# Multiplying the identity into unread PSUM columns at TensorE's waits

## The chip, the cores and the metric

The kernel runs on one core of one Trainium2 chip. The metric is the device time of that core in microseconds, the median of several runs. TensorE (PE in the profile) multiplies, VectorE (DVE), ScalarE (ACT) and GpSimd (POOL) work on SBUF and, except POOL, read PSUM; SyncE (SP) issues most of the DMAs. Each engine runs its own instruction stream in order, and they meet at semaphores. The profiler records the share of its full clock that TensorE was granted: 1.00 is 2.4 GHz, 0.50 is 1.2 GHz.

## The reference

Three parts follow each other. A delta-rule attention over 768 steps for 4 x 8 heads of 48 dimensions; a mixture of 8 experts with a greedy, capacity-bound assignment of 3072 tokens (each expert takes 384); and a dense feed-forward block with 2048 hidden units.

```python
for t in range(S):                                    # attention
    y[:, :, t] = einsum('bhd,bhde->bhe', q[:, :, t], state)
    v_old = einsum('bhde,bhd->bhe', state, kt)
    state = state + bt * einsum('bhd,bhe->bhde', kt, vt - v_old)
...
for idx in argsort(-(x @ w_gate).flatten()):          # routing
    tok, e = idx // E, idx % E
    if assigned[tok] < 0 and counts[e] < N // E: assigned[tok] = e; counts[e] += 1
...
out[mask_e] = relu(x[mask_e] @ w1[e]) @ w2[e]          # experts
h = out @ w_in;  y = (h * sigmoid(h)) @ w_out          # dense block
```

## The kernel before

Three blocks of instructions run one after the other, with a meeting of all engines between them: `constants` (identity and triangle), `attention`, `experts`.

`attention` goes through 24 tiles `n` of 128 rows (two chunks of 64 steps for 8 heads). Within a tile the triangular system is solved by a doubling scheme: `turn_k` transposes the keys, `products` forms key-key and query-key products, `level2`, `level4`, `level8` and `prod8`, `prod24` form powers of the triangle and their sum, `correct` and `apply` (three and two times) refine the right side, `read_state`, `to_state` and `outputs` exchange with the running state, and `turn_x` and `gate` transpose the output and multiply it by the gate's weights to give the routing logits. The order on TensorE is written out by hand and mixes tile `n` with `level*` and `products` of tile `n + 1` and `n + 2` and with `outputs`, `turn_x`, `gate` of tile `n - 1`. The first tile has nothing of a tile before it to mix in, and the last two tiles have less of the tiles behind them. Between these steps ScalarE and VectorE take the results out of PSUM, and GpSimd scales keys and values (`scale_k`, `scale_v`) and builds `LP` and `Hm` from the identity and the products (`unit`).

GpSimd's order matters here: `scale_k(2)`, `scale_v(2)`, and only then `unit(1)`, whose result `P1_ok` the second half of `level4(1)` waits for. `scale_v(2)` waits for the load of `v_in` for tile 2. SyncE issues that load after the two loads of 3 MB for `w_in` and `w_out`.

`experts` routes in 8 rounds. The first round has no other work to hide behind. VectorE searches the threshold in 8 steps of 4 bits (`search_digits`); in each of them TensorE counts with 24 small products (L1259), VectorE compares, TensorE spreads the hits with one product (L1262), and VectorE picks the next digit. Then `place(0, 0)` forms prefix sums, `place(0, 1..4)` turn one-hot tiles into the list of tokens, GpSimd gathers the tokens' rows of `x_rows` with three indirect DMAs, and TensorE transposes them (L1393). From there on TensorE runs the products of the experts and the dense block (`one_pass`, L1272), and the searches of the later rounds are put between them at fixed numbers of passes (L1235).

Of the kernel before, what the change touches and what calls it, by code (L numbers as in the profile page):

```python
# [14 lines left out]
C = 128  # L15
# [14 lines left out]
def by_tile(w):  # L30

    return w[:, :, :].rearrange("p a b -> p (a b)").rearrange("p (k f) -> p k f", k=KD)


def whole_and_rest(nc, sb, whole, rest, shape):
# [6 lines left out]
def attention(nc, k_t, v_t, q_t, beta_t, wg, x_rows, logits, identf, up_f, rc, PS, wi, wo, w_in, w_in_hi, w_in_lo, w_out, w_out_hi, w_out_lo):  # L42

    ctx = ExitStack()
    with ctx:
# [502 lines left out]
        def _(pe):  # L548
# [14 lines left out]
            def turn_k(n):  # L563
                pe.wait_ge(kb_ok, n + 1)
                if n:
                    pe.wait_ge(kT_sb, n)
                if n >= 2:
                    pe.wait_ge(P8_sb, n - 1)
                for i in range(HG):
                    last = nc.tensor.transpose(PS[:, 2, i * C:i * C + C], K[n % 3][:, i, :, :].rearrange("p r d -> p (r d)"), identf[:, :])  # L570
                last.then_inc(kT_ps, 1)
# [110 lines left out]
            def gate(n):  # L682
# [4 lines left out]
                    last = mm(PS[:, 7, DM:DM + E], xT[:, k, :], wg_sb[:, k, :], start=(k == 0), stop=(k == KD - 1))  # L687
                last.then_inc(lg_ps, 1)

            pe.wait_ge(mask_ok, 8)  # L690
            turn_k(0)
            products(0)
            turn_k(1)
            level2(0)
            level4(0)
            level8(0)
            products(1)
            prod8(0)
            for n in range(NT):
                nxt = n + 1 < NT  # L700
                from_state(n)
                if n:
                    outputs(n - 1)
                prod24(n)
                if n + 2 < NT:
                    turn_k(n + 2)
                correct(n, 0)
                if n:
                    turn_x(n - 1)
                apply(n, 0)  # L710
                if nxt:
                    level2(n + 1)
                correct(n, 1)
                if n:
                    gate(n - 1)
                apply(n, 1)
                if nxt:
                    level4(n + 1)
                read_state(n)
                correct(n, 2)  # L720
                if nxt:
                    level8(n + 1)
                to_state(n)
                if n + 2 < NT:
                    products(n + 2)
                if nxt:
                    prod8(n + 1)
            outputs(NT - 1)
            turn_x(NT - 1)
            gate(NT - 1)  # L730


BITS = 31
# [2 lines left out]
DIGITS = 8  # L736
# [84 lines left out]
def experts(nc, x_rows, w1, w2, w_in_hi, w_in_lo, w_out_hi, w_out_lo, out, logits, identf, up_f, rc, PS):  # L821
# [3 lines left out]
    with ctx:  # L825
# [402 lines left out]
        def _(pe):  # L1228
# [25 lines left out]
            def digits():  # L1254
                for i in range(DIGITS):
                    c0 = 0 if i == DIGITS - 1 else 1
                    pe.wait_ge(over_ok, i + 1)
                    for m in range(NT):
                        last = mm(PS[0:CANDS - c0, 3, 0:E], over[:, m, c0:CANDS], onehot[:, m, :], start=(m == 0), stop=(m == NT - 1))  # L1259
                    last.then_inc(over_ps, 1)  # L1260
                    pe.wait_ge(hits_ok, i + 1)
                    mm(PS[:, 4, 0:E], ones_b[0:CANDS - c0, :], hits[0:CANDS - c0, :], start=True, stop=True).then_inc(hits_ps, 1)  # L1262

            PLACES = 1 + NT // HOT
            AT = [17 * i + 5 * min(i, PARTS) for i in range(COUNTS)]
# [73 lines left out]
            def turn(k):  # L1339
# [26 lines left out]
                for f in range(KF2 + LAG):  # L1366
# [10 lines left out]
                    if h >= 0:  # L1377
# [6 lines left out]
                        for j in range(MT_TOK):  # L1384
                            fourth(k, j, h, 1)

            digits()
            for i in range(PLACES):
                place(0, i)
            for j in range(MT_TOK):  # L1390
                pe.wait_ge(x_ld[j], 16)
                for d in range(KD):
                    last = nc.tensor.transpose(PS[:, bank_of(("T", 0, d)), j * C:j * C + C], xg[:, j, d * C:d * C + C], identf[:, :])  # L1393
                    if j == MT_TOK - 1:
                        last.then_inc(filled, 1)
# [65 lines left out]
```

## Time and profile before

| | |
|---|---|
| median of 3 runs | 1082.27 us (1079.34 to 1089.83) |
| the profiled execution's own time | 1078.51 us |
| its span in the trace | 1076.7 us |
| PE busy (matmul) | 962.6 us, 89% of the span |
| DVE, ACT, POOL busy | 729.9, 412.4, 471.7 us |
| granted TensorE clock, mean of the records | 0.95 |

The profile is of one execution. Busy time is the time in which an engine had an instruction under way. The span is what the trace covers; the time is what the device reports for the whole launch. The granted clock has no record ahead of about 40 us in this trace, and the views show 1.00 there; the durations of the matmuls show the clock then.

### The profile page before, as it was taken

How to read it: one execution, taken by the hardware profiler on the slowest of the kernel's cores; microseconds unless marked ns; L12 is line 12 of the kernel's file. 1: busy time of each engine (PE TensorE's matmuls, PEld its weight loads, DVE VectorE, ACT ScalarE, POOL GpSimd, SP SyncE). 2: the span in 40 equal slices, each digit the busy share in tenths (PEclk: the TensorE clock that was granted, in tenths of full speed). 3: DMA queues.
4: the chain of work that ended last, by engine and by line, in shares of the span. 5: the costliest groups of instructions: out<-in, count | busy, mean ns of one | idle time of the engine just before them, and what ended most of it. 6: DMA issues, size and time to landing. Idle time of an engine off the chain costs nothing.

```text
span 1076.7 us, 32107 instructions
## 1 busy us (share of the span) xinstructions
PE 962.6 (89%) x13967; PEld 897.1 (83%) x13967; DVE 729.9 (68%) x1572; ACT 412.4 (38%) x930; POOL 471.7 (44%) x583
## 2 busy tenths in 40 slices
PE   4888889898888539989988999999999999999996
PEld 3777778887777429889987899899899899899996
DVE  5667676767665388887778788788788788783000
ACT  3444443444443034234334326326326326326321
POOL 3235545555550024345434445535535535535532
PEclk9999998999997559999998999999999999999998
DMA  8322222111110030030040030030030030030000
GB/s 294 124 70 59 66 52 59 48 48 48 47 49 18 9 139 1 1 139 23 1 140 16 9 125 23 15 126 23 15 120 28 16 118 23 23 117 23 23 1 22
DMA packets 31563, 61.93 MB, mean 58 GB/s; under 512 B 3776, under 2 KB 23360, under 8 KB 31040
## 3 DMA queue, kind: packets, MB, share of 16 engines
q1 hardware_dynamic: 28352, 50.45, 14.5%
q0 software_dynamic: 3072, 9.44, 2.7%
q8 instruction: 110, 1.80, 0.7%
q14 instruction: 29, 0.24, 0.1%
HBM read 50.44 MB, written 9.44 MB: 56 GB/s over the span
## 4 chain that ended last, share of the span: by engine, by line
PE 49%; DVE 14%; issue 1%; POOL 1%; DMA 1%; ACT 0%; DVEq 0%
PE PS L1272 47%; DVE above L1075 3%; DVE cand L1104 3%; DVE cs L1079 2%; DVE w_lo L1218 2%; PE PS L1235 1%; DVE delta L1086 1%; DMA xg<-x_rows,idx 1%; PE PS L1259 1%; PE PS L1290 1%; DVE weighed L1083 0%; DVE over L1120 0%; POOL xg L959 0%; PE PS L1250 0%; DVE w_lo L1214 0%
## 5 line engine op out<-in xcount | busy, mean ns | idle before, releaser
L952 POOL TENSOR_TENSOR act_t<-whole,act_t 128x384 fp32r<-128x384 f32 x192 | 210.6, 1100 | 303.7 <-ACT whole L1010 302.9
L1004 ACT ACTIVATE act_t<-PS 128x384 fp32r<-128x384 f32 x192 | 94.6, 492 | 376.4 <-PE PS L1272 376.4
L1272 PE MATMUL PS<-w_out_hi,act_t 128*128 128x384 f32 x768 | 222.7, 346 | 1.6 <-POOL act_t L952 1.6
L1272 PE MATMUL PS<-x2T,w_in_hi 128*128 128x384 f32 x768 | 223.3, 345 | 0.1
L1272 PEld LDWEIGHTS PS<-x2T,w_in_hi 128*128 128x128 f32 x768 | 142.2, 191 | 3.5 <-POOL x2T L952 2.0
L1272 PEld LDWEIGHTS PS<-w_out_hi,act_t 128*128 128x128 f32 x768 | 142.2, 190 | 1.9 <-POOL act_t L952 1.9
L1272 PE MATMUL PS<-w_out_lo,act_t 128*128 128x384 f32 x384 | 133.0, 346 | 0.0
L1272 PE MATMUL PS<-x2T,w_in_lo 128*128 128x384 f32 x384 | 132.0, 344 | 0.0
L1272 PE MATMUL PS<-xgT,w_hi 128*128 128x384 f32 x384 | 110.1, 346 | 0.6 <-ACT whole L1008 0.6
L1272 PE MATMUL PS<-act_t,w_hi 128*128 128x384 f32 x384 | 106.4, 337 | 0.0
L1075 DVE TENSOR_TENSOR above<-V,cand 128x576 bf16<-128x576 f32 x112 | 91.7, 818 | 3.9
L1010 ACT ACTIVATE whole<-PS 128x384 f32<-128x384 f32 x192 | 93.5, 487 | 0.0
L1079 DVE TENSOR_REDUCE cs<-above 128x24 bf16<-128x576 bf16 (+1 forms) x119 | 86.8, 730 | 4.1
L1272 PEld LDWEIGHTS PS<-w_out_lo,act_t 128*128 128x128 f32 x384 | 73.0, 190 | 0.0
L1272 PEld LDWEIGHTS PS<-x2T,w_in_lo 128*128 128x128 f32 x384 | 72.9, 190 | 0.0
L1272 PEld LDWEIGHTS PS<-xgT,w_hi 128*128 128x128 f32 x384 | 71.6, 192 | 1.3 <-DVE w_lo L1214 0.9
L1272 PEld LDWEIGHTS PS<-act_t,w_hi 128*128 128x128 f32 x384 | 69.9, 188 | 0.1
L1272 PE MATMUL PS<-xgT,w_lo 128*128 128x384 f32 x192 | 66.2, 345 | 0.0
L1272 PE MATMUL PS<-act_t,w_lo 128*128 128x384 f32 x192 | 64.9, 338 | 0.0
L656 PE MATMUL PS<-X,Hm 64*64 64x48 f32 x1536 | 61.9, 236 | 1.5 <-ACT X L303 1.1
L237 POOL TENSOR_TENSOR vs<-v_in,sqb_all 128x384 f32<-128x384 f32 x24 | 19.9, 831 | 96.6 <-DVE Bv L455 82.6
L959 POOL DMA_INDIRECT xg<-x_rows,idx x24 | 26.7, 1111 | 80.7 <-DVE idx L1211 77.9
(204 smaller groups left out, 1848.6 us busy)
## 6 DMA issues: line engine op xcount, KB each, us to landing
w_sb<-moe_w SPq DMA_DIRECT2D x16, 1536.0 KB, 8.2
k_in<-k_t SPq DMA_DIRECT2D x24, 192.0 KB, 4.2
KQ<-q_t SPq DMA_DIRECT2D x48, 96.0 KB, 2.2
v_in<-v_t SPq DMA_DIRECT2D x24, 192.0 KB, 3.1
x_rows<-ysb SPq DMA_DIRECT2D x48, 96.0 KB, 2.2
w_in<-moe_w_in SPq DMA_DIRECT2D x1, 3072.0 KB, 11.8
w_out<-moe_w_out SPq DMA_DIRECT2D x1, 3072.0 KB, 20.1
xg<-x_rows,idx POOLq DMA_INDIRECT x24, 3.1
```

Of the source, the lines that this page charges most:

```text
L237: nc.gpsimd.tensor_tensor(by_head(vs[p][:, :]), by_head(v_in[p][:, :]), sqb_all[:, n, :].unsqueeze(2).to_broadcast([C, H, D]), ALU.mult).t ...
L656: each(lambda h, b: mm(PS[rows(b), 6, col(h)], Hm[n % 2][rows(b), h, :], X[n % 2][rows(b), col(h)], start=True, stop=True)).then_inc(HX_ps, 1)
L952: nc.gpsimd.tensor_tensor(lo, whole_of(t), hi.bitcast(F32), ALU.subtract).then_inc(rest_ok, 1)
L959: nc.gpsimd.indirect_dma_start(out=xg[:, j, :], out_offset=None, in_=x_rows, in_offset=bass.IndirectOffsetOnAxis(ap=idx[k % 2][:, j:j + 1] ...
L1004: nc.scalar.activation(hi, src, func).then_inc(hi_ok, 1)
L1010: nc.scalar.activation(whole_of(t), src, func).then_inc(whole_ok, 1)
L1075: chain(v.tensor_tensor(above[:, 0:cands, :, :].rearrange("p c e m -> p c (e m)"), flat.unsqueeze(1).to_broadcast([C, cands, E * NT]), t.u ...
L1079: v.tensor_reduce(cs[:, 0:cands, :], above[:, 0:cands, :, :], AX.X, ALU.add).then_inc(cs_ok, 1)
L1086: chain(v.tensor_reduce(o, weighed[:, :, :].rearrange("p c e -> p (c e)"), AX.X, ALU.max))
L1104: v.tensor_scalar(cand[:, :], pair_i[:, i + 1, :], cur[:, 0:1], delta[:, 0:1], ALU.bitwise_xor, ALU.bitwise_xor).then_inc(dv, 1)
L1218: v.tensor_tensor(w2_part(w2_lo, q), w2_part(w2_sb, q), w2_part(w2_hi, q).bitcast(F32), ALU.subtract).then_inc(w2_split, 1)
L1272: ins = mm(o, a, b, start=start, stop=stop, skip_group_check=True)
```

## The change

`keep_busy` multiplies the identity (128 x 128, fp32) by itself into the last 128 columns of a PSUM bank, columns that nothing reads at those points. In the attention it is called with bank 5 ahead of and within the first tile, with bank 2 in the last two tiles; in the experts with bank 2 in the first routing round. No semaphore is signalled and no wait is added, and every call stands on TensorE alone, ahead of the wait of the step that follows it.

```diff
+def keep_busy(nc, PS, identf, bank, times):
+    for _ in range(times):
+        nc.tensor.matmul(PS[:, bank, 512 - C:512], identf[:, :], identf[:, :], start=True, stop=True, skip_group_check=True)
...
+            keep(5, 22)
             pe.wait_ge(mask_ok, 8)
             turn_k(0)
+            keep(5, 3)
             products(0)
             turn_k(1)
+            keep(5, 8)
             level2(0)
+            keep(5, 4)
             level4(0)
+            keep(5, 4)
             level8(0)
...
+                if n == 0:
+                    keep(5, 4)
                 prod24(n)
                 if n + 2 < NT:
                     turn_k(n + 2)
+                else:
+                    keep(2, 4)
                 correct(n, 0)
...
                 if nxt:
                     level2(n + 1)
+                else:
+                    keep(2, 3)
                 correct(n, 1)
...
                 correct(n, 2)
                 if nxt:
                     level8(n + 1)
+                else:
+                    keep(2, 2)
                 to_state(n)
...
             outputs(NT - 1)
+            keep(2, 2)
             turn_x(NT - 1)
+            keep(2, 2)
             gate(NT - 1)
+            keep(2, 6)
...  (experts; keep is keep_busy on bank 2)
                     mm(PS[:, 4, 0:E], ones_b[0:CANDS - c0, :], hits[0:CANDS - c0, :], ...).then_inc(hits_ps, 1)
+                    keep(4 if i < DIGITS - 1 else 13)
...
+            keep(10)
             digits()
             for i in range(PLACES):
                 place(0, i)
+                keep(13 if i == 0 else 2 if i < PLACES - 1 else 20)
```

## Rows read from the trace of the kernel before

**Rows 1.** The page: shares of the chain that ended last, by engine.

```profile
PE 49%; DVE 14%; issue 1%; POOL 1%; DMA 1%; ACT 0%; DVEq 0%
```

**Rows 2.** Stretches: us, busy us (instructions) of PE, PEld, DVE, ACT, POOL, clock, DMA share, GB/s.

```profile
330.60:340.80 10.20, 10.01 (x235) 9.71 (x237) 5.02 (x17) 3.79 (x11) 2.49 (x2) 0.50 0.02 4
...
347.60:360.10 12.50, 10.50 (x175) 9.51 (x175) 1.12 (x3) 2.23 (x6) 0.00 (x0) 0.50 0.07 17
360.10:396.50 36.40, 9.02 (x226) 7.10 (x226) 24.48 (x90) 4.90 (x9) 2.67 (x3) 0.50 0.26 94
396.50:405.70 9.20, 7.75 (x25) 5.95 (x26) 8.09 (x16) 4.95 (x11) 3.82 (x5) 0.50 0.13 40
```

**Rows 3.** TensorE in order of time, tiles 0 and 1: start, us, instructions.

```profile
10.87 1.08 PE L570 MATMUL PS<-identf,K 128*128 128x128 f32 x4 [10.87 <-POOL K L227]
...
36.72 0.94 PE L602 MATMUL PS<-LP,L 64*64 64x128 f16 x14
...
41.84 0.66 PE L627 MATMUL PS<-St,KQ 48*64 48x48 f32 x30
```

**Rows 4.** TensorE, tiles 21 to 23: first at clock 1.00, from 330.6 at 0.50.

```profile
316.85 0.52 PE L679 MATMUL PS<-identf,ysb 128*128 128x128 f32 x3
317.35 1.14 PE L656 MATMUL PS<-X,Hm 64*64 64x48 f32 x32
...
319.65 0.83 PE L687 MATMUL PS<-wg_sb,xT 128*128 128x8 f32 x6
...
321.64 0.56 PE L602 MATMUL PS<-LP,L 64*64 64x128 f16 x14
...
326.06 0.64 PE L627 MATMUL PS<-St,KQ 48*64 48x48 f32 x29
...
329.68 0.43 PE L647 MATMUL PS<-rb,P 64*64 64x48 bf16 x16 [0.83 <-issue]
...
330.69 1.94 PE L656 MATMUL PS<-X,Hm 64*64 64x48 f32 x32
...
342.19 0.68 PE L627 MATMUL PS<-St,KQ 48*64 48x48 f32 x32
```

**Rows 5.** One line's instructions: matmuls of turn_k, ns min/median/max.

```profile
L570 PE MATMUL PS<-identf,K x96: 272/273/473, 10.9 to 315.8; 128*128 128x128 f32 x96
```

**Rows 6.** GpSimd in order of time, behind the load of v_in for tile 2.

```profile
34.47 0.83 POOL L237 TENSOR_TENSOR vs<-v_in,sqb_all 128x384 f32<-128x384 f32 x1 [13.96 <-DMA v_in<-v_t]
35.25 1.27 POOL L246 TENSOR_TENSOR LP<-eye,GP 128x512 f16<-128x512 f32 x1
```

**Rows 7.** TensorE in the last tile, then ScalarE at the block's end.

```profile
347.66 0.62 PE L647 MATMUL PS<-rb,P 64*64 64x48 bf16 x16 [0.66 <-DVE rb L452]
348.21 1.45 PE L687 MATMUL PS<-wg_sb,xT 128*128 128x8 f32 x6
...
354.66 1.91 PE L671 MATMUL PS<-X,GP 64*64 64x48 f32 x32
...
360.11 0.34 ACT L339 COPY logits<-PS 64x8 f32<-64x8 f32 x2 [1.54 <-PE PS L687]
```

**Rows 8.** TensorE in the first routing round.

```profile
376.22 0.75 PE L1259 MATMUL PS<-onehot,over 128*15 128x8 bf16 x24 [1.22 <-DVE over L1120]
...
385.42 0.22 PE L1243 MATMUL PS<-GQ,tri 128*128 128x48 f16 x1 [3.19 <-DVE GQ L1177]
...
396.53 0.90 PE L1393 MATMUL PS<-identf,xg 128*128 128x128 f32 x3 [4.76 <-DMA xg<-x_rows,idx]
```

**Rows 9.** GpSimd at the first expert's start.

```profile
400.64 2.92 POOL L952 TENSOR_TENSOR xgT<-whole,xgT 128x384 fp32r<-128x384 f32 x3 [3.65 <-ACT whole L1008]
```

**Rows 10.** Stretches with waits and one behind a wait, columns as in Rows 2.

```profile
475.00:480.00 5.00, 2.00 (x12) 1.51 (x11) 4.86 (x6) 1.11 (x3) 3.10 (x4) 1.00 0.28 79
...
480.70:484.20 3.50, 3.50 (x13) 3.50 (x12) 3.43 (x5) 1.39 (x2) 1.67 (x1) 0.51 0.00 0
...
555.00:560.00 5.00, 3.44 (x25) 2.96 (x24) 3.96 (x9) 2.32 (x4) 3.08 (x4) 1.00 0.16 49
```

More of the change, by code:

```diff
@@ L688, in gate, with keep @@
                 last.then_inc(lg_ps, 1)
+            def keep(bank, times):
+                keep_busy(nc, PS, identf, bank, times)
+            keep(5, 22)
             pe.wait_ge(mask_ok, 8)
             turn_k(0)
+            keep(5, 3)
             products(0)
             turn_k(1)
+            keep(5, 8)
             level2(0)
+            keep(5, 4)
             level4(0)
+            keep(5, 4)
             level8(0)
@@ L1262, in digits, with keep @@
                     mm(PS[:, 4, 0:E], ones_b[0:CANDS - c0, :], hits[0:CANDS - c0, :], start=True, stop=True).then_inc(hits_ps, 1)
+                    keep(4 if i < DIGITS - 1 else 13)
+            def keep(times):
+                keep_busy(nc, PS, identf, 2, times)
             PLACES = 1 + NT // HOT
```

## The prediction

> **What bounds the kernel now.** I read the page first. Half of the chain that ended last is TensorE [rows 1], so its clock matters. The stretch view places the low clock: in this execution it lies at 0.50 from 330.6 to 340.8 and again from 347.6 to 405.7 us, that is in the last two tiles of the attention, in the whole first routing round and at the first expert's start [rows 2]. Short dips at tiles 8 to 18 are not touched by the change. The start is low too: the four transposes at 10.87 take 1.08 us [rows 3], while three take 0.52 at full clock [rows 4] and 0.90 at the low one [rows 8], and the longest of its line takes 0.47 us against a median of 0.27 [rows 5]. So it is at the low level too. In these three regions TensorE alternates between work that the clock halves and waits that it doesn't. So the reader must look, wait by wait, at two things: what a full clock saves, and whether the added products fit into the wait.
>
> **The price of one added product.** The trace has no 128 x 128 fp32 product of 128 columns. Two rows make it up. An fp32 product leaves two matmul records (three gate products are six records [rows 4]); a transpose, one record of the same shape, starts every (0.52 - 0.27) / 2 = 0.12 us at full and (0.90 - 0.47) / 2 = 0.21 us at low clock [rows 4, 5, 8], where 0.27 and 0.47 are one record's duration at each. So one call is 0.25 us at full and 0.43 us at low clock. If a plain product's record took half a transpose's, a call would be 0.12; if weight loads didn't overlap, twice the 0.25. I take 0.25 and 0.43. Everything below is what a block costs beyond the wait that it stands in.
>
> **The first tile: 0.** 22 calls start at about 2.4 us and end at 11.8 us if the clock never rises, 0.9 us after the key tile that TensorE waits for at 10.87 [rows 3]; with a rise on the way they fit. In either case it doesn't matter. What counts is the next thing that is late. GpSimd scales the values of tile 2 only at 34.47, after 13.96 us of waiting for a load that stood behind the two 3 MB loads, and builds LP of tile 1 behind that, from 35.25 to 36.52 [rows 6]; the second half of level4(1) starts at 36.72 [rows 3]. This path of DMAs doesn't know TensorE's clock. A full clock would bring TensorE to that point earlier, by about 4 us (the stretch to 36.72 is about 4.6 us of halved work), where it would wait until 36.5 all the same. Behind it, from 36.72 to from_state(1) at 41.84 are 5.12 us [rows 3], and the same steps in tile 21 take 326.06 - 321.64 = 4.42 us [rows 4]: 0.7 us are to be had, if the clock is still high after those 4 us without any product in them. Where TensorE waited for gathers (475 to 480), the clock was 0.50 right behind it [rows 10]. So I take 0, between 0.8 gained and 0.7 lost (if it now rises later than it did).
>
> **Tile 22: -2.6 us.** The four calls behind prod24(22) stand in the 0.83 us ahead of the product at 329.68 [rows 4], and the clock was at 0.50 right behind that [rows 2]. They take 0.98 us, so 0.15 too many. If they hold the clock, the stretch from apply(22, 0) to from_state(23), now 342.19 - 330.69 = 11.50 us, takes what it took a tile earlier at full clock, 326.06 - 317.35 = 8.71 us [rows 4]. That is 2.8 less 0.15. Whether the clock would have fallen there at all differs between executions; this sum is for the profiled one.
>
> **Tile 23: -2.9 us.** From the gate product at 348.21 to the end of outputs at 356.57 [rows 7] lie, at the low level, one gate (1.45 against 0.83 at full), one apply (about 1.95 against 1.14), read_state (1.1 against 0.6), one correct (0.6 against 0.4), to_state and outputs (2.8 against 1.7 together): 3.2 us less at full clock [rows 4, 7]. The 4, 3 and 2 calls ahead of the corrections and to_state are 0.98, 0.74 and 0.49 us against waits of about 0.83 (as in tile 22 [rows 4]), 0.66 [rows 7] and 0.57 us: 0.3 over. Behind outputs nothing more is won: the last output tile, copied by 357.1, must be stored by two DMAs (0.5 us each to issue, 2.2 to land), which is about 360.4, as late as the logits' copy at 360.11 to 360.45 [rows 7]. So the last 2, 2 and 6 calls (2.5 us) lie beside that store, and cost nothing unless the clock is low (then about 2).
>
> **Digits and places: +4.5 us.** Here TensorE's own work hardly depends on the clock: it waits for the end of VectorE's small steps. The gain from a full clock is at most some hundredths of a microsecond in each of 17 products. The price depends on the level. In each round TensorE waits 1.22 us between the spreading product and the next count [rows 8]. Four calls take 0.98 us at full clock, inside; at the low level 1.71, which is 0.45 to 0.5 over. Does the clock hold? The four calls are 0.98 in 2.40 us, and the 24 products of 8 columns beside them didn't lift it in the whole stretch before, though PE was busy a quarter of it [rows 2]. The nearest rows: 2.00 us of full-size work in 5 was followed by 0.50, 3.44 in 5 was not [rows 10]. 0.98 in 2.40 is 2.0 in 5, the first of them. So I take a fall in the second round, after which the share can't recover: five rounds at 0.45, or 2.2 us. The 13 calls behind the last digit are then 5.5 us in a wait of 3.19 [rows 8]: 2.1 over, since the clock rises only late in such an unbroken block. The next 13 (3.2 us) and the pairs (0.49) stand in waits for VectorE's one-hot tiles of about their own length, and the last 20 are 4.9 us against 4.76 [rows 8]; at full clock I take 0.2 for all of them. At a clock that holds, the sum of this part is -0.2; at one that never rises +13.
>
> **The first expert: -1.3 us.** The long block of 20 calls ends where the first gathered rows arrive. If the clock is high then, the last three transposes are 0.4 us shorter; but the first pass group still ends behind GpSimd's third difference, 400.64 + 2.92 = 403.56 [rows 9], so there only about 0.5 us are won. Behind it passes go at 0.17 instead of 0.32 us until 405.7, about 9 of them, 1.4 us more. The transposes leave TensorE half idle, and the clock can fall once more for a few microseconds: the ends are 0.3 and 2.0.
>
> **Sum.** 0 - 2.6 - 2.9 + 4.5 - 1.3 = -2.3 us on the profiled 1078.51 us: 1076.2. The four times shown, this one among them, have their middle at (1079.34 + 1082.27) / 2 = 1080.8, 2.3 us above the profiled one, since the executions differ in where the clock falls; the calls take away one of these places. I forecast 1077.5 us.
>
> **Rivals.**
> (a) *The calls hold the clock through the digits.* Then the part is -0.2 rather than +4.5, and the first expert keeps its 2.0: 1078.51 - 7.7 = 1070.8, with the same offset 1072. For it: no wait over 0.3 us would be left anywhere from tile 22 to the gathers. Against it: the share of busy time [rows 10]. The Trainium skill, "TensorE: Matmul & The Clock Gate", section "Why this matters for your kernels", advises to leave no long idle gaps between bursts; by that rule the digits stay fast and this rival is the outcome. The trace doesn't quite agree with the gaps as the measure: the clock fell at 330.6 behind a gap of 0.83 us [rows 4]. Chance 0.22.
> (b) *The calls run at the low clock and stand in the way, slower than before.* If the four calls in tile 22 and those in tile 23 don't hold the clock, the tiles win nothing and pay 0.9 + 0.9 + 0.6 + 0.3, the end of the block about 2, the digits 7 x 0.48 = 3.4 and 2.3, the places about 1, less 1 at the expert: some +9, so 1088 to 1090. It decides from the point where a call costs 0.43 instead of 0.25 in the digit rounds while the tiles gain nothing. Chance 0.1.
> (c) *The change does nothing.* The clock isn't moved by these products (no row of the trace shows it moved by any such), but they are shorter than I price them and fit into the waits: 1079 to 1082. Chance 0.13.
> (d) *More instructions.* Some 130 calls are about 520 more instructions for TensorE, and the trace shows stalls that nothing explains ("issue"), 1% of the chain [rows 1]. A new one of 1 to 2 us in a tile would take half of the forecast's gain; it stays within the range. Chance 0.05; the rest, 0.5, is the forecast.
>
> **How the numbers follow.** The forecast alone spans 1073 to 1081 (its unknown ends: 1.5 at the start, 1.7 at the expert, 3 in the digits, and the spread of executions). To hold 8 in 10 the range must take in most of (a) and of (c) and part of (b): 1069 to 1087. A change of 1%, about what a measurement of this kernel can tell from none, is 10.8 us. Faster by that needs less than 1071.5, half of (a) and a tail of the forecast: 0.12. Slower by that needs over 1093, a tail of (b): 0.03. Within 1%: 0.85.
>
> **What would show it.** Right: matmuls of tile 0 at full-clock durations, and yet level4(1)'s second half near 36.6 us behind the same DMA; clock 1.00 from tile 22 on, with from_state(23) 8.7 us behind apply(22, 0); digit rounds of 2.4 us while the clock is high and 2.8 to 2.9 after it has fallen; the wait for GQ gone; clock 1.00 at the first transposes. Wrong: digit rounds of 2.35 us at clock 1.00 throughout (rival a); a record of the added products over 0.2 us apart at full clock; or a shorter start, if the load of tile 2's values isn't what ends the wait there.

## The result and the profile after

| | before | after |
|---|---|---|
| median, 20 runs each | 1082.78 us | 1090.01 us |
| lowest and highest | 1078.69, 1089.83 | 1081.55, 1101.33 |
| the profiled execution's own time | 1078.51 us | 1092.40 us |
| its span | 1076.7 us | 1090.7 us |
| PE busy | 962.6 us | 1006.1 us |

The ratio after to before, both run in turn on one chip, is 1.0053, with a 95% interval of 1.0031 to 1.0074: about 5.8 us slower (0.0053 x 1082.78). This leaves out the run of 1101.33 us, which fell into a slower state, and goes by all other runs, so it differs from the 7.2 us between the two medians. I had forecast 1077.5 us and a range up to 1087, so the time lies outside the range.

The shares of the chain that ended last are the same percentages as before [rows 1], although TensorE is busy for 43.5 us more. Some of that fills waits, and some of it is a longer run at the low clock. The page of after, its chain by engine:

```profile
PE 49%; DVE 14%; POOL 1%; issue 1%; DMA 1%; ACT 0%; DVEq 0%
```

I cut both profiles at the same instructions; where one stage ends the next begins. All in us, to a tenth:

| stage | before | after | forecast change |
|---|---|---|---|
| start to from_state(1) | 41.8 | 43.4 | 0 |
| from_state(1) to from_state(22) | 284.2 | 298.0 | none made |
| tile 22 | 16.2 | 12.2 | -2.6 |
| tile 23 to VectorE's first routing step | 18.6 | 15.6 | -2.9 |
| routing to the first expert product | 39.9 | 44.8 | +4.5 |
| first 48 expert products of 384 columns | 11.1 | 12.7 | -1.3 |
| the rest | 665.0 | 664.0 | none made |

Two things stand out. The five stages that I had summed come to +1.1 us in these two profiles (+1.6 - 4.0 - 3.0 + 4.9 + 1.6) instead of -2.3. And 13.8 of the 14.0 us by which the two spans differ lie in tiles 1 to 21, where the change adds nothing.

**The start.** TensorE in after's trace in order of time (start, duration, instructions, and in brackets the idle time before them with its releaser), to be read beside [rows 3]:

```profile
2.45 6.72 PE L38 MATMUL PS<-identf 128*128 128x128 f32 x44 [2.45 <-PEq L1433]
10.95 0.63 PE L576 MATMUL PS<-identf,K 128*128 128x128 f32 x4 [1.77 <-POOL K L233]
...
37.13 0.96 PE L608 MATMUL PS<-LP,L 64*64 64x128 f16 x14 [4.10 <-POOL LP L252]
...
43.43 0.66 PE L633 MATMUL PS<-St,KQ 48*64 48x48 f32 x30
```

The 44 records (22 calls) are over at 9.2, the four transposes take 0.63 us instead of 1.08, and TensorE is early, as forecast. It then waits 4.10 us for LP. GpSimd gives that at the same point as before [rows 6]:

```profile
35.02 0.83 POOL L243 TENSOR_TENSOR vs<-v_in,sqb_all 128x384 f32<-128x384 f32 x1 [15.17 <-DMA v_in<-v_t]
35.81 1.26 POOL L252 TENSOR_TENSOR LP<-eye,GP 128x512 f16<-128x512 f32 x1
```

GpSimd goes on 0.55 us later (35.02 against 34.47), and the clock is low behind the wait, so 43.43 stands against 41.84.

**Tiles 22 and 23.** The stretch that was at 0.50 [rows 2, 4] is at full clock, and the meeting of the engines comes 0.30 us behind the last added product. TensorE in order of time, then the stretch view (from:to, us, busy us and instructions of PE, PEld, DVE, ACT and POOL, granted clock, DMA share, GB/s):

```profile
355.39 1.16 PE L38 MATMUL PS<-identf 128*128 128x128 f32 x8
356.48 0.43 PE L653 MATMUL PS<-rb,P 64*64 64x48 bf16 x16
...
366.64 0.84 PE L693 MATMUL PS<-wg_sb,xT 128*128 128x8 f32 x6
367.33 1.58 PE L38 MATMUL PS<-identf 128*128 128x128 f32 x12
369.21 2.47 PE L38 MATMUL PS<-identf 128*128 128x128 f32 x20 [0.30 <-PEq L51]
```

```profile
353.60:369.20 15.60, 14.89 (x344) 13.41 (x345) 3.93 (x7) 3.99 (x12) 0.00 (x0) 1.00 0.12 28
369.20:377.80 8.60, 6.85 (x100) 6.05 (x101) 5.47 (x21) 0.20 (x1) 0.00 (x0) 1.00 0.01 3
377.80:398.30 20.50, 19.01 (x202) 17.21 (x198) 8.93 (x39) 0.00 (x0) 0.00 (x0) 0.50 0.02 3
```

**Digits.** The last two of these stretches are the first routing round. The clock holds to 377.8 and then lies at 0.50 for 20.5 us. TensorE in order of time:

```profile
375.06 0.75 PE L1284 MATMUL PS<-onehot,over 128*15 128x8 bf16 x24 [0.64 <-DVE over L1145]
376.06 0.17 PE L1287 MATMUL PS<-hits,ones_b 15*128 15x8 bf16 x1 [0.25 <-DVE hits L1149]
376.17 1.16 PE L38 MATMUL PS<-identf 128*128 128x128 f32 x8
377.45 0.75 PE L1284 MATMUL PS<-onehot,over 128*15 128x8 bf16 x24
378.45 0.18 PE L1287 MATMUL PS<-hits,ones_b 15*128 15x8 bf16 x1 [0.25 <-DVE hits L1149]
378.56 2.08 PE L38 MATMUL PS<-identf 128*128 128x128 f32 x8
380.57 0.75 PE L1284 MATMUL PS<-onehot,over 128*15 128x8 bf16 x24
381.57 0.18 PE L1287 MATMUL PS<-hits,ones_b 15*128 15x8 bf16 x1 [0.25 <-DVE hits L1149]
381.68 2.08 PE L38 MATMUL PS<-identf 128*128 128x128 f32 x8
383.69 0.75 PE L1284 MATMUL PS<-onehot,over 128*15 128x8 bf16 x24
...
394.16 5.12 PE L38 MATMUL PS<-identf 128*128 128x128 f32 x26
```

The same four calls (8 records) take 1.16 us at full and 2.08 at the low clock. A round, from one count to the next, is 377.45 - 375.06 = 2.39 us at full clock and 3.12 at the low one (380.57 to 383.69). The count itself, 24 products of 8 columns, takes 0.75 at both: it doesn't know the clock. And at the low clock the wait for VectorE's `over`, which was 1.22 us [rows 8], is gone: the added products are now what the count waits for. Between the meeting and the fall at 377.8 no idle time of TensorE is longer than 0.64 us.

**The first expert.** The clock rises at 398.3, at the end of the 13 calls behind the last digit, and holds through the places. But the gathers then come one by one, and it falls once more at 415.3:

```profile
411.52 0.55 PE L1424 MATMUL PS<-identf,xg 128*128 128x128 f32 x3 [0.73 <-DMA xg<-x_rows,idx]
412.68 0.55 PE L1424 MATMUL PS<-identf,xg 128*128 128x128 f32 x3 [0.61 <-DMA xg<-x_rows,idx]
```

```profile
411.90:415.30 3.40, 1.72 (x11) 0.97 (x9) 3.21 (x5) 2.26 (x6) 1.31 (x2) 1.00 0.05 19
415.30:422.20 6.90, 6.63 (x21) 5.97 (x22) 3.98 (x9) 1.88 (x5) 3.90 (x4) 0.51 0.00 0
```

### The profile page after: what moved, and what is told of

Read it like the earlier page. It is cut to its first block, busy times and chain, and to the rows that moved or that the text cites. A ratio compares the mean times of both kernels' runs of the same rounds, so it can differ in the third digit from the quotient of the medians.

```text
span 1090.7 us, 32739 instructions
## 1 busy us (share of the span) xinstructions
PE 1006.1 (92%) x14283; PEld 938.6 (86%) x14283; DVE 729.1 (67%) x1572; ACT 412.8 (38%) x930; POOL 472.5 (43%) x583
## 4 chain that ended last, share of the span: by engine, by line
PE 49%; DVE 14%; POOL 1%; issue 1%; DMA 1%; ACT 0%; DVEq 0%
PE PS L1301 46%; DVE above L1100 3%; DVE cand L1129 3%; DVE cs L1104 2%; DVE w_lo L1243 2%; PE PS L38 1%; PE PS L1260 1%; DVE delta L1111 1%; DMA xg<-x_rows,idx 1%; PE PS L1284 1%; PE PS L1319 1%; DVE weighed L1108 0%; POOL xg L984 0%; PE PS L1275 0%; DVE w_lo L1239 0%
## 5 line engine op out<-in xcount | busy, mean ns | idle before, releaser
L662 PEld LDWEIGHTS PS<-X,Hm 64*64 64x64 f32 x1536 | 56.4, 152 | 8.4 <-ACT X L309 7.3
```

The costliest lines, as they stand in the source:

```text
L662: each(lambda h, b: mm(PS[rows(b), 6, col(h)], Hm[n % 2][rows(b), h, :], X[n % 2][rows(b), col(h)], start=True, stop=True)).then_inc(HX_ps, 1)
```

## The experiments

There were four studies, each with its own runs of the kernel before on the same chip, whose medians were 1085.35, 1081.53, 1077.78 and 1084.28 us. Times are compared within a study only, by the ratio given with its 95% interval. "Profiled" stages are those of the table above.

### One region at a time (first study)

**e1_front**: before with the 45 calls around the first tile alone.

```diff
 before
+            keep(5, 22)
...
+                if n == 0:
+                    keep(5, 4)
```

> Only the 45 calls in and ahead of the first tile; the last tiles and the routing are as before. Theory A (the start costs): TensorE waits some 4 us for LP of tile 1, the clock falls in that wait and comes back 3 us later than it did, so from_state(1) is 1 to 2 us late, and the 180 instructions more move the places at which the instruction stream stalls in tiles 1 to 21, which costs up to 3 us more: 1.5 to 4.5 us over before. Rival B (the start only moves work inside a wait): within 1 us of before, and the loss of the whole change lies in the routing.

Measured 1087.37 us, ratio 1.0006 (0.9976 to 1.0036): no change that can be told, so rival B's outcome and not the loss of theory A. from_state(1) came at 42.7 instead of 41.8. Tile 22, in which this kernel has no call, took 11.8 us, since the clock did not fall there; the 4.0 us that after gains in it are thus not shown to be the calls' work.

**e2_tail**: before with the calls of tiles 22 and 23 and behind the last outputs alone (`keep(2, ...)` in the attention).

```diff
 before
+                else:
+                    keep(2, 4)
...
+            gate(NT - 1)
+            keep(2, 6)
```

> Only the 23 calls in the last two tiles and behind outputs. Both theories: the clock holds at 1.00 from tile 22 to the end of the attention, and the time is 3 to 5 us under before; digit rounds of 2.40 us. If the calls at the end stand in the way of the meeting of the engines, about 1 us of it is lost.

Measured 1083.17 us, ratio 0.9993 (0.9961 to 1.0024). In the profile tiles 22 and 23 are 2.0 and 3.0 us shorter (14.2 and 15.6), as their clock is high; in the median of 12 runs only 0.8 us of that is seen, with an interval of 3.4 us to either side. The 3 to 5 us that I had expected here did not come.

**e3_routing**: before with the calls of the first routing round alone.

```diff
 before
+                    keep(4 if i < DIGITS - 1 else 13)
...
+            keep(10)
             digits()
             for i in range(PLACES):
                 place(0, i)
+                keep(13 if i == 0 else 2 if i < PLACES - 1 else 20)
```

> Only the calls of the first routing round. Theory A and B both price the digits: rounds of 2.4 us at full clock and 3.1 at the low one, some 5 us in all, and 1 to 2 more at the first expert, whose clock falls while the gathers land: 5 to 7 us over before. If instead the first expert starts at full clock, 3 to 4 us over.

Measured 1093.5 us, ratio 1.0064 (1.0038 to 1.0089): 6.9 us slower, the whole loss of the change and a little more. Its routing stage is 48.6 us in the profile against 39.9.

**e4_align**: the whole change, with 19 small products ahead of the first added call, so that the instructions added ahead of the tiles' loop and in tile 0 (45 calls of 4, and 76) come to 256. TensorE's stalls that the trace calls "issue" repeat every 256 instructions (below), and the rival was that the shifted code stalls at worse points.

```diff
 after
+def pad_small(nc, PS, identf, bank, times):
+    for _ in range(times):
+        nc.tensor.matmul(PS[0:16, bank, 504:512], identf[:, 0:16], identf[:, 0:8], start=True, stop=True, skip_group_check=True)
...
+            pad_small(nc, PS, identf, 5, 19)
             keep(5, 22)
```

> The whole change, with 19 small products more (76 instructions, 16 x 8 columns) ahead of the 22 calls, where TensorE waits in any case, so that the first tile's calls add 256 instructions and not 180. Theory A: the stalls of the instruction stream in tiles 1 to 21 fall on the same steps as in the kernel before, and the time is 1 to 3 us under that of the whole change. Rival (the stalls don't sit at every 256th instruction, or where they fall is of no weight): the same time as the whole change within 1 us.

Measured 1092.11 us, ratio 1.0049 (1.0012 to 1.0086), as the change itself. The stalls of tiles 1 to 21 sum to 22.1 us as in after, so the place of the code among the blocks of 256 isn't what makes them, and the 1 to 3 us that the shift was to give back did not come. Its profile shows something else: tile 23 took 24.0 us instead of 15.6, most of it at clock 0.50, with all added products in it. TensorE in order of time and the stretch view:

```profile
352.77 0.38 PE L597 MATMUL PS<-P,L 64*64 64x64 f16 x13 [1.51 <-issue]
...
357.62 1.65 PE L38 MATMUL PS<-identf 128*128 128x128 f32 x6
```

```profile
353.90:371.00 17.10, 16.91 (x241) 15.40 (x241) 2.10 (x4) 3.20 (x8) 0.00 (x0) 0.50 0.05 11
```

A stall of 1.51 us came first, and then TensorE stayed at 0.50 for 17.1 us, busy as it was (16.91 of them). That the stall brought the fall is likely and not shown: in e16 a stall of 1.50 us stands ahead of a fall at the same point, but in after one of 1.59 us just ahead of tile 22 (until 341.04) is followed by full clock. The search then began at full clock, and four blocks of four calls ran at it before it fell at 388.0, where after had two.

### How many products a digit bears, and the late load (second study)

**e5_digits0**: the whole change without the calls in the digit rounds and ahead of them.

```diff
 after
-                    keep(4 if i < DIGITS - 1 else 13)
...
-            keep(10)
```

> The whole change without the calls inside the digit search and the 10 ahead of it; the calls from the first place on stay. Theory A (the digits' calls overrun their waits once the clock is low, and the share of work they bring can't hold it): digit rounds of 2.40 us at either level, GQ's product 4 to 6 us sooner behind the search's start than in the whole change, and the time 4 to 5 us under it. Rival (the loss of the routing lies in the place blocks): rounds of 2.40, but the stretch from the routing's start to the first pass stays over 43 us.

Measured 1080.68 us, ratio 1.0008 (0.998 to 1.0036): the loss is gone. The rounds are back at 2.40 us, with the wait of [rows 8] in them again. The 13 calls behind the first place, at clock 0.50 all through, take 5.89 us where the wait is 3.15, which leaves the stage at 41.1:

```profile
377.43 0.75 PE L1284 MATMUL PS<-onehot,over 128*15 128x8 bf16 x24 [1.22 <-DVE over L1145]
...
386.71 5.89 PE L38 MATMUL PS<-identf 128*128 128x128 f32 x26
```

**e6_digits6**: six calls instead of four in each of the first seven rounds.

```diff
 after
-                    keep(4 if i < DIGITS - 1 else 13)
+                    keep(6 if i < DIGITS - 1 else 13)
```

> The whole change with 6 calls in each digit round and not 4. Theory A: at full clock the 12 records take 1.6 us in a wait of 1.22, so rounds are about 2.8 us, but the clock holds through the search, and the 13 calls behind it fit: the search with its blocks takes about what it takes with 4 calls, and less than with 4 in an execution that fell early. If the clock falls all the same, rounds of 4.1 us and 7 us more than the whole change.

Measured 1082.94 us, ratio 1.0038 (1.0003 to 1.0072). TensorE in order of time and the stretch from the meeting to 400 us, into the search's end:

```profile
377.59 0.75 PE L1284 MATMUL PS<-onehot,over 128*15 128x8 bf16 x24
...
378.69 1.60 PE L38 MATMUL PS<-identf 128*128 128x128 f32 x12
380.23 0.75 PE L1284 MATMUL PS<-onehot,over 128*15 128x8 bf16 x24
```

```profile
369.20:400.00 30.80, 28.57 (x376) 25.91 (x374) 19.79 (x73) 3.31 (x5) 2.07 (x2) 1.00 0.31 107
```

The clock is 1.00 throughout. Six calls at full clock cost 0.24 us a round beyond the wait (2.64 against 2.40), four at the low clock 0.72 (3.12). More added work makes a shorter stage in this profile, 41.3 us against 44.8: the price of the digits hangs on the clock first, and on the number of calls second. It is one profile, and the time is still above that of the kernel before.

**e7_vload**: before with the values of tile 2 loaded ahead of the two loads of 3 MB.

```diff
 before
+            load_v(2)
             sp.dma_start(by_tile(w_in)...)
...
-                if n + 2 < NT:
+                if n and n + 2 < NT:
```

> The kernel before, with the load of the values of tile 2 ahead of the two 3 MB loads and not behind them; no call is added. Theory A (two things are late together at tile 1's level4: LP, behind that load, and TensorE at the low clock): LP is there 15 us earlier, and still from_state(1) starts within 0.7 us of where it did (41.8), so the same time. Rival (the load alone is the bound): from_state(1) 2 us or more earlier.

Measured 1077.52 us, ratio 0.9979 (0.9944 to 1.0014): in time no change that can be told. In the profile the wait for the load is gone, GpSimd goes on at 27.62 and from_state(1) comes at 38.4 instead of 41.8. I had expected nothing from the load alone; the rival, 2 us or more at from_state(1), came. GpSimd, then TensorE:

```profile
27.62 0.83 POOL L238 TENSOR_TENSOR vs<-v_in,sqb_all 128x384 f32<-128x384 f32 x1 [7.10 <-DVE Bv L456]
...
33.91 0.94 PE L603 MATMUL PS<-LP,L 64*64 64x128 f16 x14
38.45 0.65 PE L628 MATMUL PS<-St,KQ 48*64 48x48 f32 x30
```

**e8_vload_front**: e7 and the 45 calls of e1.

```diff
 e7_vload
+            keep(5, 22)
...
+                if n == 0:
+                    keep(5, 4)
```

> The same earlier load, with the 45 calls of the first tile. Theory A: now nothing holds level4 of tile 1, the 4 us wait for LP is gone, the clock doesn't fall in it, and from_state(1) starts 4 to 6 us earlier than before (36 to 38), which is what the calls were worth if the load had not stood in the way. Rival (the calls at the start are worth nothing in any case): from_state(1) at 41 to 43.

Measured 1079.74 us, ratio 0.9985 (0.9952 to 1.0017). from_state(1) at 40.4, later than with the load alone. The theory by which the calls pay once the load is out of the way asked for 36 to 38 and missed, as did the rival with its 41 to 43: the clock fell at 27.2 for 13.7 us in spite of the calls. In all eight profiles with these 45 calls it fell between 26 and 30, and in e3, e7 and e9, which don't have them, at 28.4 or 28.5.

### The earlier load with the calls of the last two tiles (third study)

**e9_vload_tail**: e7 and the calls of e2.

```diff
 e7_vload
+                else:
+                    keep(2, 4)
...
+            gate(NT - 1)
+            keep(2, 6)
```

> The earlier load of tile 2's values, and only the 23 calls of the last two tiles. Theory A (these two are what is to be won): from_state(1) near 38.4 and the last tile with the block's end 3 us shorter unless a stall of the instruction stream meets it: 4 to 6 us under before. Rival (the last tiles' calls are worth nothing on the average, as their own run of 12 suggested): 2 to 3 us under.

Measured 1070.13 us over 6 runs, ratio 0.9903 (0.987 to 0.9935). Its profile, of an execution of 1076.86 us, has from_state(1) at 38.7 and tiles 22 and 23 at 12.7 and 16.2 us.

**e10_vload_tail_hold**: e9, and behind it only as many calls as fit the waits from the last digit to the gathers.

```diff
 e9_vload_tail
+                    if i == DIGITS - 1:
+                        keep(5)
...
+                keep(6 if i == 0 else 1 if i < PLACES - 1 else 18)
...
+                keep(3 if j < MT_TOK - 1 else 2)
```

> The same, and routing calls sized to fit at the low clock (0.5 us each): none in the first 7 digit rounds, 5 behind the last, 6, 1, 1, 1 and 18 at the places, and 3, 3 and 2 between the transposes of the gathered rows, in bank 7. Theory A: digit rounds 2.40, the search with its places as long as before, the clock 1.00 at the first expert, whose first 48 passes take 9 to 9.5 us and not 11.1: 1 to 2 us under the kernel without these calls. Rival (the first expert is bound by ScalarE's and GpSimd's splits and not by the clock): the first 48 passes take over 10.5 us at clock 1.00.

Measured 1070.44 us over 8 runs, ratio 0.9918 (0.9884 to 0.9952): as e9. The 1 to 2 us that its calls were to win can't be told. The calls, here in bank 7, did give full clock at the first expert, which is what was tried. The stretch view and TensorE there:

```profile
392.00:402.20 10.20, 9.50 (x51) 8.21 (x52) 8.86 (x18) 4.40 (x11) 6.31 (x6) 1.00 0.01 2
```

```profile
395.00 0.62 PE L1296 MATMUL PS<-xgT,w_hi 128*128 128x384 f32 x2 [0.51 <-POOL xgT L971]
```

The 48 products took 10.2 us instead of 11.1, more than the 9 to 9.5 of theory A and less than the rival's 10.5. So a full clock over the whole of it is worth at most some 0.9 us: one wait of 0.51 us for GpSimd's split stands inside it, and e2 and e16, with no added product in the routing, took 10.5 too.

**e11_fit_low**: the whole change with the calls cut down so that they fit their waits even at the low clock.

```diff
 after
-                    keep(4 if i < DIGITS - 1 else 13)
+                    keep(2 if i < DIGITS - 1 else 6)
...
-                keep(13 if i == 0 else 2 if i < PLACES - 1 else 20)
+                keep(6 if i == 0 else 1 if i < PLACES - 1 else 20)
```

> The whole change, with 2 calls in each digit round and not 4, and 6 and not 13 in the two long waits, which fit at 0.5 us each. Theory A (the routing's loss is the overrun at the low clock): rounds of 2.40 us at the low clock, and from the routing's start to the first pass 39.5 to 41 us as before, not 43 to 49: 4 to 5 us under the whole change, equal to before within 2. Rival (it is something else that the added products do to VectorE's chain): rounds over 2.5.

Measured 1078.17 us, ratio 0.9993 (0.9963 to 1.0023). The routing stage is 39.8 us, as before the change, and the loss is gone. Two calls (4 records) at the low clock just fit between the start of such a block and the next count, 375.58 to 376.87. TensorE, and the clock there:

```profile
375.58 1.22 PE L38 MATMUL PS<-identf 128*128 128x128 f32 x4
376.87 0.75 PE L1284 MATMUL PS<-onehot,over 128*15 128x8 bf16 x24
```

```profile
373.00:380.00 7.00, 6.21 (x87) 5.03 (x87) 3.51 (x15) 0.00 (x0) 0.00 (x0) 0.50 0.00 0
```

**e12_again**: the kernel before, unchanged, to see how far two profiles of one program lie apart.

> The kernel before once more, unchanged. Theory A (in tiles 1 to 21 the clock falls at other places in each execution, and the profiled one was a short one): its tiles 1 to 21 take 289 to 298 us and not 284.2, and its time is that of before within 0.3%. Rival (the added instructions lengthen these tiles): 283 to 286 again.

Measured 1077.33 us, ratio 0.9986 (0.9959 to 1.0012). Its tiles 1 to 21 took 286.3 us against 284.2, with 34.4 instead of 20.5 us of low clock in them. That is under the 289 to 298 of theory A; it takes e2, e3 and e15 below to show that the same code also takes 292 to 297 us.

### The loss by itself, and once more (fourth study)

**e13_front_tail**: the whole change without the routing calls.

```diff
 after
-                    keep(4 if i < DIGITS - 1 else 13)
...
-            keep(10)
...
-                keep(13 if i == 0 else 2 if i < PLACES - 1 else 20)
```

> The whole change without any call in the routing. Theory C (the routing carries the loss; start and end together win a little): 0 to 4 us under before, 5 to 7 us under the whole change; 16 to 20 us of stalls of the instruction stream in tiles 1 to 21. Rival A (the first tile's calls lengthen the tiles behind them through more such stalls, 20 us or more): 1 to 4 us over before.

Measured 1083.92 us, ratio 0.9993 (0.9961 to 1.0025): within theory C's 0 to 4 us under before, and without rival A's loss. Its stalls in tiles 1 to 21 sum to 17.5 us.

**e14_routing_again**: e3, unchanged.

> Only the routing calls, the same kernel as in the first study of them. Theory C: 5 to 8 us over before again; the stretch from the routing's start to the first pass 44 to 49 us. Stalls in tiles 1 to 21 of 16 to 20 us.

Measured 1090.92 us, ratio 1.0075 (1.0047 to 1.0104): 8.1 us slower, with a routing stage of 47.8 us. The stalls came to 21.4 us and not 16 to 20. The clock is low when the stage begins, and then the 10 calls ahead of the search cost too:

```profile
362.25 4.61 PE L38 MATMUL PS<-identf 128*128 128x128 f32 x20 [0.69 <-PEq L51]
366.79 0.75 PE L1268 MATMUL PS<-onehot,over 128*15 128x8 bf16 x24
```

The first count starts 4.54 us behind the meeting. In after, where the same calls ran at full clock, it starts 2.95 us behind it (369.21 to 372.16).

**e15_digits_only**: before with the four calls in the first seven digit rounds and nothing else.

```diff
 before
+                    keep(4 if i < DIGITS - 1 else 0)
```

> The kernel before with 4 calls in each of the first 7 digit rounds, and nothing else. The clock is low when the search begins, since nothing has held it. Theory C (a call is 0.5 us at the low level, four are 2.0 in a wait of 1.22): rounds of 3.12 us throughout and 7 x 0.72 = 5.0 us over before. Rival (four calls in each round lift the clock by themselves): rounds of 2.4 after the first ones, under 2 us over before.

Measured 1089.8 us, ratio 1.0045 (1.0011 to 1.0079), routing stage 44.4 us, which is 4.5 more: the first block stands in a longer wait, 1.73 us in before, and costs 0.2, the other six 0.72 each. TensorE in order of time:

```profile
377.46 0.75 PE L1268 MATMUL PS<-onehot,over 128*15 128x8 bf16 x24
378.46 0.18 PE L1271 MATMUL PS<-hits,ones_b 15*128 15x8 bf16 x1 [0.25 <-DVE hits L1133]
378.58 2.08 PE L38 MATMUL PS<-identf 128*128 128x128 f32 x8
380.58 0.75 PE L1268 MATMUL PS<-onehot,over 128*15 128x8 bf16 x24
```

A round is 3.12 us at a clock that stays at 0.50 for the whole stage: four calls a round didn't lift it here, as they didn't hold it in after. These 28 calls alone cost 0.45%, against 0.64 and 0.75% for all calls of the routing and 0.53% for the whole change.

**e16_best_again**: e9, unchanged.

> The earlier load and the calls of the last two tiles again. Theory: 0.6 to 1.1% under before (its first runs said 0.97), from_state(1) at 38 to 42. If that was luck of the executions, 0.3% or less.

Measured 1080.67 us over 12 runs, ratio 0.9979 (0.9949 to 1.0009). By what I had written, the 0.97% of the first six runs was in the main luck of the executions. In this profile the clock fell in tile 23 although the added products were there, and that tile took 22.9 us; from_state(1) came at 38.2. So e9 was faster in both studies, by 10 us in one and by 2 in the other as the ratios say, and the second interval includes no change. Both exclude a loss of more than 0.1%; how much faster it is, if at all, isn't shown.

## Why the prediction was wrong

**Two terms of the sum failed.** Measured alone, the calls of the routing cost 6.9 and 8.1 us (e3, e14); I had summed +4.5 - 1.3 = +3.2 for them, which lies outside both intervals. The calls of tiles 22 and 23 gained 0.8 us alone (e2) and 0.8 together with those of the start (e13); I had summed -5.5, outside both intervals too. The two misses, some 4 to 5 us each, make up the distance between the forecast change of -3.3 us (1077.5 against 1080.8) and the measured +5.8. Most of the rest is the base: the kernel before had its median at 1082.8 and not 1080.8.

**Digits and places, +4.5 us: too small.** The mechanism was right: the calls are inside their waits at full clock and outside them at the low one, and four of them don't hold the clock. Even the price per record was: 4 records take 1.22 us at the low clock (e11) and 8 take 2.08, so (2.08 - 1.22) / 4 = 0.215 us each, where I had 0.21 from transposes; at full clock 8 take 1.16 and 12 take 1.60, 0.11 each against my 0.12. What was mis-sized is the block: each pays some 0.3 us once (1.22 - 4 x 0.215 = 0.36), whatever its number of calls, which I had left out. I had 1.71 us for four calls, and the next count starts 2.01 us after them (378.56 to 380.57). The block has 1.28 us (376.17 to 377.45), so it is 0.72 over and not 0.45 to 0.5, and the round is 3.12 us instead of the 2.8 to 2.9 forecast.

Five such rounds cost 3.6 us in after (2.2 forecast), seven blocks 4.5 in e15. In after the 13 calls behind the last digit cost 1.7 us more (GQ's product starts 6.07 us behind the last count, 4.37 before; 2.1 forecast), and the places are 0.4 shorter (0.2 longer forecast). So the stage came to +4.9, and that this is near my +4.5 is partly luck of the parts and partly of the execution: the clock came out of the attention full and fell only at the third round's block, not in the second. Where it comes out low, the stage costs +7.9 and +8.7 (e14, e3), and in e14 the 10 calls ahead of the search make 1.6 of it, which the +4.5 doesn't have. How long four calls hold the clock differs as well: four blocks in e4 (whose stage cost +3.6), two in after, one in e14, none in e15.

**First expert, -1.3 us: wrong sign.** I had the second fall of the clock as one end, "0.3", and not as a loss. It was +1.6 in after, and 10.7 to 12.8 us against 11.1 in the profiles with routing calls like these: the transposes come in pieces with waits of 0.6 to 0.7 us between them, PE was busy for 1.72 of 3.40 us, and the clock was 0.51 for the next 6.9. The rows had shown just that, 2.00 us of work in 5 followed by a fall [rows 10]. I used them for the digits and not here. e10 shows what there was to win at all: 0.9 us, and not the 2 that I had as an end.

**The start, 0: right about the bound, short on the consequence.** The wait for LP is there (4.10 us, "about 4" was forecast) and 0.7 was one of the ends. The clock had fallen at 29.6, 3.4 us before this wait begins, among waits of 0.3 to 0.6 us, and stayed low through it:

```profile
29.60:43.30 13.70, 8.84 (x232) 8.45 (x234) 3.60 (x6) 3.00 (x6) 4.10 (x4) 0.50 0.38 127
```

That is +1.6 us in this profile and 0.9 in e1's, but not a loss that is shown: over the profiles with the load in its old place, from_state(1) comes at 41.9 to 43.4 with the calls (seven, 42.5 on average) and at 41.1 to 42.7 without (six, 42.1). The DMA is the bound, and e7 shows it the positive way: taken away, from_state(1) comes 3.4 us earlier without one added product. With e7's load the calls still gave nothing (e8). Why the clock falls at 26 to 30 us with them and without is open; waits and a stall stand there and no call. In e10, with e7's load and no calls at the start, from_state(1) came at 42.3 behind a stall of 2.00 us at 28.2, so the 3.4 us are not in every execution.

**Tiles 22 and 23, -2.6 and -2.9 us: there in this profile, gone in the median.** In the two profiles they are -4.0 and -3.0. Of the first, not all is the calls' doing: in e1 and e8, without a call in it, tile 22 took 11.8 us, less than the 12.2 of after. The last six calls and the logits' copy were in balance, as forecast: the meeting is 0.30 us behind the last product. But that is where the clock stays up. e4 and e16 are executions where it doesn't, and there tile 23 takes 24.0 and 22.9 us against 18.6 before. In the medians e2 shows 0.8 us for the calls of both tiles, not 5.5. The kernel before, for its part, doesn't have its low clock there in each execution either; I had written so, and then summed for the one that I saw. That is the step that failed here. Over all profiles the two tiles take 30.0 us on average with their calls (ten profiles, 27.3 to 37.9) and 33.4 without (eight, 30.4 to 35.8): a gain is likely, but its size is not what one pair of profiles says.

**The term that I had not made: tiles 1 to 21.** I set my sum against the profiled 1078.51 us and added 1.3 us of the 2.3 by which the other executions lay above it. In fact the code in these tiles, the same instruction for instruction, gave 284.2, 286.3, 288.2, 292.5, 295.9 and 297.2 us in six profiles of kernels that differ only behind them (before, e12, e14, e3, e15 and e2). The profile that I worked from was the shortest of the six. All 18 profiles fit 259.1 us + 0.34 x (us of low clock) + 1.07 x (us of stalls), to within 1.6 us. By this fit 9.4 us between the two profiles come from the clock (47.8 against 20.5 us of it low) and 6.5 from stalls (22.1 against 16.0), 15.9 together for 13.8 measured. A single profile thus can't price a change of 5 us in this kernel. What it can do is show the mechanism at one place. The fit says what goes together and not what makes the clock fall.

**Adding up.** By stages of single profiles: routing +4 to +9, the start about 0 to +1.6, the first expert -0.4 to +1.7, the two tiles down to -7 where they hold and nothing or worse where they don't. The measured +5.8 is inside, but such a sum is too wide to prove it. The experiments say it more sharply: routing alone 1.0064 and 1.0075, everything but routing 0.9993. So the loss is the routing calls', shown twice, and the four calls per digit are much of it (1.0045; without the digits' calls 1.0008, with two of them and shorter blocks 0.9993).

**What stays open.** The eight profiles that have the 45 calls of the first tile show stalls of 21.0 us in tiles 1 to 21 on average and 293.2 us for those tiles; the ten without them 18.5 and 289.9. The difference, 3.3 us, is well within what single profiles scatter (281 to 298). The medians of e1, e8 and e13 leave room for 3 us either way. That the front calls have any effect behind the first tile is not shown, nor excluded.

**Of the rivals**, (b) named the mechanism that decided, added products at the low clock standing in the way, but asked that the tiles gain nothing and was priced at +9; in the digits it is what happened, in the medians the tiles gained nothing that can be told either, and I gave it 0.1. That the measured 1090.0 is just its "1088 to 1090" is part luck: its listed terms add up to 10.4 and not 9, and the measured change is +5.8. Rival (a) is refuted for four calls and came true for six in e6's one profile, at a price that it left out: a digit then costs 0.24 us at full clock. The rule of the Trainium skill behind it ("TensorE: Matmul & The Clock Gate", section "Why this matters for your kernels") asks for no long gaps; in the digits of after no gap was longer than 0.64 us, and the clock fell. Rival (d), new stalls, is the open point above; its count was low, since the change has 158 calls and 632 instructions (32739 on the page of after against 32107), not 130 and 520.

## What to carry to other kernels

A block that is added into a wait must fit it at the low clock, its fixed part included, for that is where it runs when it fails to hold the clock. If it holds the clock only at a size that overfills the wait, leave it out. Ask first what the wait waits for: here moving one load brought from_state(1) some 3 us forward in three profiles of four, and 45 products did not. And where the time of untouched code scatters by more than the change is worth, sum the terms against several profiles, not against one.

## What the runs showed of the hardware

A busy TensorE isn't a fast one. In after PE was busy for 19.01 of 20.50 us of the search (93%) at clock 0.50, in e6 for 28.57 of 30.80 (93%) at 1.00, with the same counts of 8 columns between four calls in the one and six in the other. The busy share of the profile doesn't tell which level a stretch gets.

TensorE stalls in a pattern. In tiles 1 to 21 the idle times of 0.3 us and more (the longest is 1.95) that the trace gives to "issue" all stand at position 193 to 195 of TensorE's records, matmuls and weight loads counted together, modulo 256. They stand mostly at every third such place, in every kernel. Two of before's and one of after's:

```profile
55.95 0.61 PE L627 MATMUL PS<-St,KQ 48*64 48x48 f32 x26 [1.00 <-issue]
...
313.29 0.38 PE L580 MATMUL PS<-KQ 48*64 48x128 f32 x3 [1.28 <-issue]
```

```profile
58.18 0.84 PE L677 MATMUL PS<-X,GP 64*64 64x48 f32 x21 [1.10 <-issue]
```

The Trainium skill, "Runtime: NRT & Kernel Launch", section "Instruction fetch mechanics", says that instructions are fetched in blocks of 256, and that crossing from one to the next is mostly hidden. The spacing agrees with the traces. "Hidden" does not: they sum to 15 to 27 us over 21 tiles, on an engine whose instructions here are short (32 products start within about 1.1 us [rows 4]). Whether the fetch is the cause was not tried beyond e4, in which a shift of the code changed nothing.
